# Output gate of a gated linear-attention and mixing kernel: Sigmoid on ScalarE against exp(-o) on ScalarE with one wide reciprocal on VectorE

## The reference, cut to what matters

```python
for t in range(S):
    m_new = np.maximum(f[t] + m, i[t])
    C = exp(f[t] + m - m_new) * C + exp(i[t] - m_new) * outer(v[t], k[t])
    n = exp(f[t] + m - m_new) * n + exp(i[t] - m_new) * k[t]
    denom = np.maximum(np.abs(n @ q[t]), 1.0)
    o = 1.0 / (1.0 + np.exp(-o_gate[t]))
    y[t] = o * (C @ q[t]) / denom
h = relu(x.T @ w_tok1) @ w_tok2      # x is y with the heads side by side
u = x + h.T
out = u + relu(u @ w_ch1) @ w_ch2
```

## Time and profile before

| | |
|---|---|
| median of 3 runs | 469.45 us (467.89 to 469.51) |
| the profiled execution | 467.59 us |
| its span, first to last instruction | 465.9 us |
| granted TensorE clock | 1.000 of full speed |
| PE busy | 442.2 us, 95% of the span |
| DVE busy | 264.2 us, 57% |
| ACT busy | 228.9 us, 49% |

### The profile page before, as it was taken

The page is one execution under the profiler, slowest core; times in us unless marked ns, Lnnn a source line. Parts: engine busy times, 40 slices in busy tenths (PEclk is TensorE's granted clock), DMA queues, the critical chain, the costliest instruction groups (busy, mean ns, idle before and its releaser), DMA issues.

```text
span 465.9 us, 9523 instructions
## 1 busy us (share of the span) xinstructions
PE 442.2 (95%) x3471; PEld 408.0 (88%) x3471; DVE 264.2 (57%) x592; ACT 228.9 (49%) x570; POOL 176.8 (38%) x239
## 2 busy tenths in 40 slices
PE   6999989699999998999999998999999998999996
PEld 2577978589999997899999997899999997999996
DVE  6889964677766537666675227466685325222212
ACT  4665447657666247766653227966663113211111
POOL 6625410567665232676662203466663000000000
PEclk9999999999999999999999999999999999999999
DMA  7556990143444412444454012444410010000101
GB/s 210 195 156 185 348 267 30 37 123 118 138 135 153 135 46 86 138 139 138 127 161 127 13 42 85 135 128 137 139 59 1 2 42 1 0 2 0 44 1 42
DMA packets 36520, 47.38 MB, mean 102 GB/s; under 512 B 3324, under 2 KB 28986, under 8 KB 36474
## 3 DMA queue, kind: packets, MB, share of 16 engines
q1 hardware_dynamic: 35674, 45.79, 32.3%
q10 hardware_dynamic: 800, 0.98, 0.7%
HBM read 42.73 MB, written 4.03 MB: 100 GB/s over the span
## 4 chain that ended last, share of the span: by engine, by line
PE 80%; ACT 7%; DVE 5%; issue 4%; DMA 2%; SPq 1%; POOL 0%; DVEq 0%; ACTq 0%
PE pC L1155 31%; PE pA L1226 6%; PE pA L1227 6%; PE pA L1228 6%; PE pS L1067 6%; PE pA L1155 4%; PE pY L1124 4%; PE pA L1231 3%; PE pA L1230 3%; PE pY L1103 2%; PE pN L1079 2%; ACT gb L608 1%; PE pA L1185 1%; DMA u<-i_gate_dram 1%; DMA qz<-qT_dram 1%
## 5 line engine op out<-in xcount | busy, mean ns | idle before, releaser
L976 DVE SCALAR_TENSOR_TENSOR h_lo<-pA,h_hi 128x384 fp32r<-128x384 f32 x96 | 53.3, 555 | 133.1 <-ACT h_hi L758 133.1
L758 ACT ACTIVATE h_hi<-pA 128x384 fp32r<-128x384 f32 x96 | 46.7, 486 | 127.2 <-PE pA L1231 127.2
L1155 PE MATMUL pC<-wc_hi,h_hi 128*128 128x320 f32 x288 | 94.1, 327 | 0.8 <-DVE wc_lo L843 0.7
L1155 PE MATMUL pC<-wc_lo,h_hi 128*128 128x320 f32 x288 | 88.7, 308 | 0.0
L1155 PE MATMUL pC<-wc_hi,h_lo 128*128 128x320 f32 x288 | 88.4, 307 | 0.0
L490 POOL TENSOR_TENSOR gb<-gb,pb 128x384 f32<-128x384 f32 (+1 forms) x54 | 48.2, 893 | 81.9 <-ACT pb L618 81.9
L1226 PE MATMUL pA<-uT_hi,wc_hi 128*128 128x384 f32 x192 | 65.2, 340 | 1.9 <-DVE uT_hi L954 1.9
L1227 PE MATMUL pA<-uT_lo,wc_hi 128*128 128x384 f32 x192 | 64.7, 337 | 0.0
L1228 PE MATMUL pA<-uT_hi,wc_lo 128*128 128x384 f32 x192 | 64.4, 335 | 0.0
L1155 PEld LDWEIGHTS pC<-wc_hi,h_hi 128*128 128x128 f32 x288 | 54.0, 188 | 2.1 <-DVE h_lo L976 1.0
L1155 PEld LDWEIGHTS pC<-wc_lo,h_hi 128*128 128x128 f32 x288 | 54.2, 188 | 0.1
(11 more groups left out here) (128 smaller groups left out, 882.1 us busy)
## 6 DMA issues: line engine op xcount, KB each, us to landing
gb<-g_dram SPq DMA_DIRECT2D x18, 512.0 KB, 3.9
kv<-kvN_dram SPq DMA_DIRECT2D x24, 324.0 KB, 3.5
kd<-kT_dram SPq DMA_DIRECT2D x24, 180.0 KB
qz<-qT_dram SPq DMA_DIRECT2D x72, 60.0 KB
out_dram<-u SPq DMA_DIRECT2D x24, 160.0 KB, 1.9
qd<-qT_dram SPq DMA_DIRECT2D x20, 180.0 KB, 2.6
gq<-g_dram SPq DMA_DIRECT2D x45, 60.0 KB
wc_raw<-w_ch_dram SPq DMA_DIRECT2D x6, 384.0 KB, 5.3
```

The source lines that it names most:

```text
L758: nc.scalar.activation(h2[0][:, slot % 2], pA[slot % 2][:, 0:HALF], ACT.Relu).then_inc(h2_hi, 1)
L976: nc.vector.scalar_tensor_tensor(h2[1][:, slot % 2], pA[slot % 2][:, 0:HALF], 0.0, h2[0][:, slot % 2].bitcast(F32), ALU.max, ALU.subtract) ...
L1155: ins = mm(dst, a[p], b[q], start=first and n == 0, stop=last and n == 2)
```

## The change

The Sigmoid becomes Exp with a scale of -1, so that `x` holds exp(-o). In `values`, DVE makes the denominator as before from two small instructions, then (1 + exp(-o)) times the denominator for all 320 numbers in one instruction, its reciprocal over 320 numbers, and last the product with the numerator in PSUM. The small reciprocal over 8 numbers and one multiplication of 320 go, an addition with multiplication of 320 and a reciprocal of 320 come. The numerator is now read by the last instruction of the chain, so PE waits for `x_ready` where it waited for `y_read` and `y_den`. The first gate's DMAs wait in ACT's queue until the two gate rows have landed.

```diff
-            def sigmoid(b):
+            def o_exps(b):
                 for half in range(2):
                     act.wait_ge(o_in[half], 16 * (b + 1))
-                nc.scalar.activation(x[:, :, :], x[:, :, :], ACT.Sigmoid).then_inc(so_ready, 1)
+                nc.scalar.activation(x[:, :, :], x[:, :, :], ACT.Exp, scale=-1.0).then_inc(o_exp, 1)
 
             o_tiles = o_gate[0, :, :].rearrange("(c p) d -> p c d", p=L)
+            act.wait_ge(gates_in, 32)
             for i, (first, last) in enumerate(O_PARTS):
                 act.dma_start(x[:, first:last], o_tiles[:, first:last]).then_inc(o_in[i], 16)
-            sigmoid(0)
+            o_exps(0)
...
-                nc.vector.tensor_tensor(xc, num[:, :, 0:D], x[:, c].rearrange("p (h d) -> p h d", h=H),
-                                        ALU.mult).then_inc(y_read, 1)
                 nc.vector.tensor_scalar_max(den[:, :], num[:, :, D], 1.0).then_inc(y_den, 1)
-                dve.wait_ge(y_den, 3 * n + 1)
-
+                dve.wait_ge(y_den, 2 * n + 1)
                 nc.vector.scalar_tensor_tensor(den[:, :], num[:, :, D], -1.0, den[:, :], ALU.mult,
                                                ALU.max).then_inc(y_den, 1)
-                dve.wait_ge(y_den, 3 * n + 2)
-                nc.vector.reciprocal(den[:, :], den[:, :]).then_inc(y_den, 1)
-                dve.wait_ge(y_den, 3 * n + 3)
-                dve.wait_ge(y_read, n + 1)
-                nc.vector.tensor_tensor(xc, xc, den[:, :].unsqueeze(2).broadcast_to([128, H, D]),
-                                        ALU.mult).then_inc(x_ready, 1)
+                dve.wait_ge(y_den, 2 * n + 2)
+
+                nc.vector.scalar_tensor_tensor(xc, xc, 1.0, den[:, :].unsqueeze(2).broadcast_to([128, H, D]),
+                                               ALU.add, ALU.mult).then_inc(x_whole, 1)
+                dve.wait_ge(x_whole, n + 1)
+                nc.vector.reciprocal(xc, xc).then_inc(x_turned, 1)
+                dve.wait_ge(x_turned, n + 1)
+                nc.vector.tensor_tensor(xc, num[:, :, 0:D], xc, ALU.mult).then_inc(x_ready, 1)
...
                 if g == 0 and gone > 0:
 
-                    pe.wait_ge(y_read, gone)
-                    pe.wait_ge(y_den, 3 * gone - 1)
+                    pe.wait_ge(x_ready, gone)
```

More of the change, by code:

```diff
@@ L55 @@
 BEHIND = 3
-SECOND_SIGMOID_AT = 2
+SECOND_O_AT = 2
 SECOND_AT = 3
@@ L206, in program @@
         w_lo = sem("w_lo")
-        so_ready = sem("so_ready")
+        o_exp = sem("o_exp")
         e_exp = sem("e_exp")
@@ L227, in program @@
         y_den = sem("y_den")
-        y_read = sem("y_read")
+        x_whole = sem("x_whole")
+        x_turned = sem("x_turned")
         x_ready = sem("x_ready")
@@ L761, in batch @@
                             split_hi(n)
-                    if more and slot == (SECOND_SIGMOID_AT if b == 0 else 0):
-                        sigmoid(b + 1)
+                    if more and slot == (SECOND_O_AT if b == 0 else 0):
+                        o_exps(b + 1)
                     if more and step_in(b, slot) >= -1:
@@ L897, in values @@
                 dve.wait_ge(y_mm, STEPS * ba + NG * (c + 1))
-                dve.wait_ge(so_ready, ba + 1)
+                dve.wait_ge(o_exp, ba + 1)
                 if n != 0:
```

## The result

The changed kernel takes 546.33 us (median of 6 runs, 543.67 to 550.49), the kernel before 469.21 in the same comparison. The ratio is 1.165, with a 95% interval of 1.161 to 1.170: 77 us slower. Forecast were 523 us and a range of 504 to 540; the direction is right, the time lies outside the range.

A forecast was written before the change was run, and what follows sets the result against it. PE, busy 95% of the span, was taken as the bound, with DVE also tight in batch 0's attention. Terms -4.4 + 44.5 + 12.3 + 0.5 + 0.5 = +53.4 gave 523 us on the median's scale, range 504 to 540.

The forecast's parts named there:

- rival 4: In the slots: granted clock falls to half for the slot behind each stall, 60 us on top, 583 us; chance 0.05.
- signs of being wrong: Named beforehand: a RECIPROCAL of 0.5 us, 3 us stalls at L1103 with shorter slots behind, or a granted clock under 1.
- table loads: At the gates of batches 1 to 3: removed loads give back -2.6 and -1.8, in all -4.4 us.
- the start: First gate's DMAs behind the gate rows: bounds -1.9 and +3 us, taken as +0.5.
- batch 0: Batch 0's attention: six `values` 2.2 us longer each, 13.4 us, of which 1.1 is covered: +12.3 us.
- 15 waits for the bank, and the ends of batches: PE's stalls at chunk changes in batches 1 to 3, +44.5 us, and last `values` of batches, +0.5 us.
- The price of R: DVE's reciprocal over 320 numbers: surplus of 43 to 63 ns read as per number, 1.88 to 2.66 us, taken as 2.3.
- Rivals 1 and 2: DVE's wide reciprocal: eight plain slopes a number, 2.80 us, 533, chance 0.22; or fixed surcharge, 0.53 us, 485, chance 0.11.
- The new wait: PE waits for the bank at 15 chunk changes: 10.0 us plus 15 times the wide reciprocal's time, +44.5 us.
- rival 3: In the slots: PE makes up each stall before the next chunk, 465 us, faster by 4.4; chance 0.02.
- Nothing counted for what DVE has late: Steady slots: PE needs DVE's late L976 and L853 only some 3.5 us after its release, so no cost counted.
- rival 2: DVE's wide reciprocal: the surplus is a fixed surcharge, 0.53 us, so +15.8 us in all, 485 us; chance 0.11.

The follow-up runs named there:

- fillers: Matmuls on constants in PE's idle time, results never read: added to the changed kernel, 520.45 us; added for batch 0 and start to the wide-reciprocal-in-batch-0 kernel, 481.39 us.
- Tanh kernel: Kernel before with the gate as (1 + tanh(o/2))/2, no wide reciprocal and one table load: 462.65 us, ratio 0.988.
- the two Tanh kernels: Kernel before with the tanh gate, 462.65 us, and the same with the first gate's DMAs waiting for the gate rows, 464.67 us.
- wide reciprocal in batch 0 alone: Kernel before with tanh gate and late first gate, but batch 0 has the change's Exp gate and `values`, PE waiting for `x_ready` there: 486.31 us, ratio 1.040.
- Tanh with the late gate: Kernel before with the tanh gate, and the first gate's DMAs waiting for the two gate rows: 464.67 us, ratio 0.992.
- The release alone: Kernel before with PE waiting for `x_ready` in place of `y_read` and `y_den`, DVE's work unchanged: 480.12 us, ratio 1.025.

## Why the prediction was wrong

**The direction and the mechanism of the wait were right; the step that failed is the dismissal of rival 4, the clock.** I gave it 0.05, because an idle of 2.84 us before the change had left the clock at 1.00. One stretch of that length doesn't stand for 15 of 2.5 to 4 us, 13 of which were followed by a fall, and for a batch 0 in which PE is idle 4.4 of 10 us; a clock under 1 was also one of my signs of being wrong. What sets the waits with a fall apart from those without one stays open. The rival's price was wrong as well: I put a full slot at half clock behind each stall, 60 us; the trace has about 3 us at half clock and 1.5 us lost, and 26 us in all with batch 0's share. With the clock held up by fillers the kernel takes 520.45, within 3 us of the forecast. That it comes so close is in part luck: some terms below are off in opposite directions, and the fillers leave the clock at 0.986.

Term by term. The kernels form a chain, each compared with the next, so the measured column adds up to the whole by construction, but for the difference between the comparisons' own medians; it proves nothing by adding up. One term is good to 1 or 2 us:

| term | forecast | measured | how |
|---|---|---|---|
| table loads | -4.4 | -5.5 | Tanh kernel less before |
| the start | +0.5 | +2.0 | the two Tanh kernels |
| batch 0 | +12.3 | +21.6 | wide reciprocal in batch 0 alone, less Tanh with the late gate |
| 15 waits for the bank, and the ends of batches | +45.0 | +60.0 | the changed kernel less wide reciprocal in batch 0 alone |
| sum | +53.4 | +78.1 | directly measured: 77.1 |

- **The price of R**, read from 8 numbers: 2.3 forecast, 2.15 measured. Reading the surplus of 43 to 63 ns as a price per number was right. Rivals 1 and 2 fall with it.
- **The new wait**: 10.0 + 15 x 2.15 = 42.3 forecast with the true R; 41.4 measured, 39.5 of it new. The release alone gave 9.9 new where the same working gave 11.2. That PE gives nothing back (rival 3) was right. The row's 60.0 are 18 us beyond 42.3, and 13 falls of the clock at 1.5 us are 20; the differences of medians are no finer than that.
- **Batch 0**: the 12.3 counted DVE's queue at PE's full speed. At least 4.9 of the missing 9.3 us are the clock by the medians. By the traces it is more: with fillers the second layer of token mixing is 12.4 us late, near the 12.3, and without them 22.2. The fillers leave some slow stretches there, so this closeness is partly chance too.
- **The start**: the value of 0.5 was too small. With one table load, as in the changed kernel, the move costs 2.0, within the bound of +3; in the changed kernel itself its price can't be told from the times. I had counted ACT's lateness, not that PE stands 2.4 us behind it and that the clock falls there as well (0.79 from 12 to 20 us).
- **Table loads**: 2.84 + 0.91 + 0.86 of idle went in full, 4.6 in all, where I had taken 2.57 of the first. By the traces each gate gave 0.1 to 0.3 us more than its idle, 5.2 in all; the last 0.3 lies within the runs' spread. The 1.28 us a load without a drain behind it carried the sum well.
- **Nothing counted for what DVE has late**: right for the changed kernel only, where PE itself stands still in front of the bank. Once the bank is free, the same 2.15 us cost 1.7 us a chunk through three short waits.
- **Slips in the working**: six times 2.22 us is 13.3, not 13.4; rival 2's sum leaves out the 0.5 for the ends of batches; and rival 3's 465 leaves out batch 0's 12.3, which a PE that makes up the slots' stalls would not give back, so it should have been 477. None of them moves the forecast or its range noticeably.

## What to carry to other kernels

Price an operation's slope from the smallest row if there is no other, but look at what the last read of a shared PSUM bank stands behind: moving a long instruction in front of it puts its full length on PE.
## What the runs showed of the hardware

- A wait of 3.99 us on TensorE was followed by 3 us at near half the granted clock (0.54 from 124.80 to 128.30 us); one of 2.71 us was followed by 0.57 from 240.40 to 244.40. Of the 15 waits of 2.5 to 4 us, 13 were followed by such a fall and two were not (1.00 behind 307.11 and 416.05). Waits of 0.2 to 0.6 us, three times in 14.3 us, left it at 1.00.
- In batch 0 the clock fell behind two waits of 2.04 and 2.37 us and stayed at half for some 34 us while PE was busy without a gap from 42 us on, and rose at 76.7 us, within token mixing.
- RECIPROCAL on DVE: 152 ns and 6.25 ns a number, float32 in SBUF, 320 numbers in 2153 ns in all 24 instances, within 2 ns.
